# A diagonal of r·u·k made on VectorE in token order, in a linear-attention, MLP and soft-expert kernel

## What is computed

```python
# r, k, v, w: (batch 4, heads 8, seq 768, head_dim 48); u: (8, 48)
for t in range(S):
    kt, vt, rt, wt = (k[:, :, t], v[:, :, t], r[:, :, t], w[:, :, t])
    cur = np.einsum('bhd,bhe->bhde', u[None] * kt, vt)
    y[:, :, t] = np.einsum('bhd,bhde->bhe', rt, state + cur)
    state = wt[:, :, :, None] * state + np.einsum('bhd,bhe->bhde', kt, vt)
...
h = x @ w_in                                  # x: 3072 x 384, w_in: 384 x 2048
x = (h * (1.0 / (1.0 + np.exp(-1.702 * h)))) @ w_out
# then soft experts: phi 384 x 32, 8 experts, w1 384 x 1024, w2 1024 x 384 each
```

## Time and profile before

| | |
|---|---|
| time, median of 3 runs | 597.43 us (597.21 to 599.02) |
| profiled execution, its own time | 598.29 us |
| span of its trace | 596.6 us |
| granted TensorE clock, mean | 0.992 |
| PE busy | 573.4 us (96%), 6335 instructions |
| DVE busy | 329.6 us (55%) |
| ACT busy | 264.0 us (44%) |
| chain that ended last | PE 83%, DMA 7%, DVE 3%, issue 3%, ACT 2%, SP's queue 2% |

### The profile page before, as it was taken

The page is one execution under the profiler, slowest core; times in us unless marked ns, Lnnn a source line. Parts: engine busy times, 40 slices in busy tenths (PEclk is TensorE's granted clock), DMA queues, the critical chain, the costliest instruction groups (busy, mean ns, idle before and its releaser), DMA issues.

```text
span 596.6 us, 15329 instructions
## 1 busy us (share of the span) xinstructions
PE 573.4 (96%) x6335; PEld 523.4 (88%) x6335; DVE 329.6 (55%) x713; ACT 264.0 (44%) x540; POOL 10.5 (2%) x28
## 2 busy tenths in 40 slices
PE   8889999999999999999999999999999999999983
PEld 6788989889989998999999999999999999998332
DVE  8778777657846664566445645576364224323304
ACT  3955444363463335333544344333533356554313
POOL 4010000000000000000000000000000000000000
PEclk9999999999999999999999999999999999999996
DMA  8994523323432322222212322232111197768728
GB/s 282 381 221 161 150 79 102 90 79 89 110 97 73 87 70 63 63 66 84 87 50 87 88 57 78 73 88 73 56 48 27 40 387 243 230 223 280 245 77 317
DMA packets 52983, 77.52 MB, mean 130 GB/s; under 512 B 4256, under 2 KB 33440, under 8 KB 52576
## 3 DMA queue, kind: packets, MB, share of 16 engines
q1 hardware_dynamic: 41872, 54.88, 28.8%
q10 hardware_dynamic: 10240, 18.50, 10.1%
q0 software_dynamic: 800, 3.15, 1.7%
HBM read 67.46 MB, written 9.04 MB: 128 GB/s over the span
## 4 chain that ended last, share of the span: by engine, by line
PE 83%; DMA 7%; DVE 3%; issue 3%; ACT 2%; SPq 2%; ACTq 0%; DVEq 0%
PE hps L1417 33%; PE acc L1552 32%; DMA spare<-w_in 4%; DMA w2s<-w 2%; PE zps L1340 2%; PE mps L1358 2%; PE yps L1352 1%; PE mps L1451 1%; PE mps L1635 1%; PE zps L1352 1%; PE mps L1668 1%; PE zps L1346 1%; DMA out<-obuf 1%; PE mps L1648 1%; PE hps L1712 1%
## 5 line engine op out<-in xcount | busy, mean ns | idle before, releaser
L1185 DVE TENSOR_TENSOR gl<-g,gh 128x384 fp32r<-128x384 f32 (+1 forms) x144 | 73.9, 513 | 209.0 <-ACT gh L865 208.9
L1417 PE MATMUL hps<-xh,wi_hi 128*128 128x384 f32 (+1 forms) x432 | 146.8, 340 | 3.5 <-ACT g L854 2.2
L1417 PE MATMUL hps<-xh,wi_lo 128*128 128x384 f32 (+1 forms) x432 | 137.2, 318 | 0.0
L1417 PE MATMUL hps<-xl,wi_hi 128*128 128x384 f32 (+1 forms) x432 | 137.0, 317 | 0.0
L854 ACT ACTIVATE g<-hps 128x384 f32<-128x384 f32 (+1 forms) x144 | 65.6, 455 | 146.4 <-PE hps L1417 146.2
L1552 PE MATMUL acc<-wo_hi,gl 128*128 128x384 f32 x384 | 129.2, 337 | 0.0
L1552 PE MATMUL acc<-wo_lo,gh 128*128 128x384 f32 x384 | 129.2, 336 | 0.0
L1552 PE MATMUL acc<-wo_hi,gh 128*128 128x384 f32 x384 | 129.0, 336 | 0.2 <-issue 0.2
L865 ACT ACTIVATE gh<-g 128x384 fp32r<-128x384 f32 (+1 forms) x144 | 70.5, 489 | 118.1 <-PE acc L1552 117.5
L1417 PEld LDWEIGHTS hps<-xh,wi_hi 128*128 128x128 f32 x432 | 81.2, 188 | 13.7 <-issue 5.3
L1417 PEld LDWEIGHTS hps<-xl,wi_hi 128*128 128x128 f32 x432 | 81.5, 189 | 0.9
(11 more groups left out here) (251 smaller groups left out, 734.2 us busy)
## 6 DMA issues: line engine op xcount, KB each, us to landing
w1s<-w SPq DMA_DIRECT2D x16, 768.0 KB, 6.6
w2s<-w SPq DMA_DIRECT2D x16, 768.0 KB, 6.2
raw<-dmaj ACTq DMA_DIRECT2D x40, 225.8 KB, 2.6
vn<-vnat SPq DMA_DIRECT2D x24, 192.0 KB, 2.5
tests<-wall SPq DMA_DIRECT2D x6, 768.0 KB, 15.0
out<-obuf SPq DMA_DIRECT2D x12, 384.0 KB, 4.0
raw<-dmaj ACTq DMA_DIRECT2D x20, 226.2 KB, 2.5
raw<-dmaj ACTq DMA_DIRECT2D x20, 225.3 KB, 2.5
```

The lines of the kernel that those rows point to most:

```text
L1185: dve.tensor_tensor(out=gl[F % 2][:, 0:wide], in0=g32[F % 2][:, 0:wide], in1=gh[F % 2][:, 0:wide].bitcast(fp32), op=ALU.subtract).then_inc ...
L1417: last = pe.matmul(hps[F % 2][:, 0:wide], w[:, g, at:at + 128], v[i % 2][:, g, 0:wide], start=m == 0, stop=m == 3 * G - 1)
```

## The change

The bonus no longer goes through PE for n of 2 and more. r and k come a second time in token order (rknat, one load per block by ACT's queue, `load_n`, in place of the load of v's field; the first, for block 2, by SP), and v's field leaves raw. DVE's `weigh(n)` multiplies r·k, multiplies by u (u_row), and sums each head's 48 numbers: three instructions that wait for one another, giving b as a column of 8 numbers per token. `mask_scores(n)` first writes b times an identity (eye) over all of `scores` and then copies the PE scores over it where the mask is set, so the block's own output matmuls add b·v. The outputs then need no sum: ACT copies them from zps and yps to ybuf (`take_output`), for n = 0 and 1 DVE does (`first_output`). For n = 0 and 1 b still comes from PE, in matmuls with 2 columns. In the slot tables weigh stands at one slot where bonus_a and bonus_b were, some parts of blocks 2 to 4 move by a slot, and low_part(4) moves from slot 6 to behind the meeting of slot 5. SP issues raw 2 after the products of block 0 and not after bonus_values(0).

```diff
-        raw = [sb(f"raw{i}", [R, 4, HP, C + 1]) for i in range(2)]
+        raw = [sb(f"raw{i}", [R, NQ, HP, C + 1]) for i in range(2)]
...
-        ruk = [sb(f"ruk{i}", [R, HP, C]) for i in range(2)]
-        rukh = sb("rukh", [R, HP, C], f32r)
-        rukl = sb("rukl", [R, HP, C], f32r)
...
+        natural = sb("natural", [C, 2, DM])
+        u_row = sb("u_row", [C, DM])
+        bonus = [sb(f"bonus{i}", [C, H]) for i in range(2)]
...
-        place_parts(2, scan=1, invert=1, grow=2, decayed=3, bonus_a=4, turn=4, bonus=6)
-        place_parts(3, scan=5, invert=7, grow=7, turn=8, decayed=8, bonus_a=8, bonus=10)
-        place_parts(4, scan=13, invert=14, grow=15, turn=16, decayed=15, bonus_a=11, bonus_b=13, split=16, bonus=17)
...
+        place_parts(2, scan=1, invert=1, grow=2, weigh=3, decayed=3, turn=4, mask=8)
+        place_parts(3, load_n=5, scan=5, invert=6, grow=6, decayed=7, turn=8, weigh=9)
+        place_parts(4, load_w=7, load_k=9, load_r=10, load_n=11, scan=13, invert=14, grow=15, weigh=14, decayed=15, turn=16)
...
             n, f = BASE[i + 1] + 1, NF * i
-            place_parts(n, scan=f - 6, invert=f - 5, grow=f - 5, bonus_a=f - 3, bonus_b=f - 2, decayed=f - 1,
...
-            place_parts(n + 1, scan=f + 1, invert=f + 2, grow=f + 3, bonus_a=f + 4, bonus_b=f + 4, decayed=f + 5,
-                        turn=f + 5, split=f + 5, bonus=f + 6, load_w=f - 2, load_k=f - 1, load_r=f, load_v=f + 1)
+            place_parts(n, load_w=f - 8, load_k=f - 7, load_r=f - 6, load_n=f - 5, scan=f - 6, invert=f - 5, grow=f - 5,
+                        weigh=f - 2, decayed=f - 1, turn=f)
+            place_parts(n + 1, load_w=f - 2, load_k=f - 1, load_r=f, load_n=f + 1, scan=f + 1, invert=f + 2, grow=f + 3,
...
-        low_at = {0: 2, 4: 3, 6: 4, 9: 5, 10: 6, 12: 7}
+        low_at = {0: 2, 4: 3, 9: 5, 10: 6, 12: 7}
+        low_behind = {5: 4}
...
             for n in range(NCH):
                 if n < PRE:
-                    sp.wait_ge(uv_done, n + 1)
+                    sp.wait_ge(decayed_done, n + 1)
+                    sp.wait_ge(front, n + 1)
+                    sp.wait_ge(rk_made, n + 1)
                     load_raw(n + 2)
+                if n == 0:
+                    sp.dma_start(u_row[:, :], urow).then_inc(u_row_in, 16)
+                if n == 1:
+                    sp.dma_start(natural[:, :, :], rknat[PRE]).then_inc(rows_in, 16)
...
                 act.activation(kn[n % 2][:, :, :], mps[:, 0:HP * R].rearrange("t (p d) -> t p d", p=HP),
                                ACT.Copy).then_inc(kn_done, 1)
 
+            def take_output(n):
+
+                act.wait_ge(meetings, met_out[n])
+                if n >= 2 * PRE:
+                    act.wait_ge(y_stored[n % 2], 32 * (n // 2 - 1))
+                else:
+                    act.wait_ge(permuted, PRE)
...
+                    cols = slice(HALF * c, HALF * (c + 1))
+                    last = act.activation(ybuf[n % 2][:, :, cols], (zps, yps)[c][0:R, 0:HP * HALF].rearrange("e (p t) -> e p t", p=HP),
+                                          ACT.Copy)
...
-                if (F, "load_v") in part_at:
-                    n = part_at[F, "load_v"]
-                    act.wait_ge(uv_done, n - 1)
...
-                if (F, "split") in part_at:
-                    n = part_at[F, "split"]
...
-                    act.activation(rukh[:, :, :], ruk[n % 2][:, :, :], ACT.Copy).then_inc(rukh_done, 1)
+                if (F, "load_n") in part_at:
+                    n = part_at[F, "load_n"]
+                    act.wait_ge(weighed, 3 * (n - PRE))
+                    act.dma_start(natural[:, :, :], rknat[n]).then_inc(rows_in, 16)
                 if (F, "turn") in part_at:
                     turned_keys(part_at[F, "turn"])
+                if F in meeting_at and meeting_at[F][0] is not None:
+                    take_output(meeting_at[F][0])
...
-
-                if n == FULL and half == 0:
-                    dve.wait_ge(u_in, 16)
-                await_field(n, RR)
-                await_field(n, KK)
-                for p in (2 * half, 2 * half + 1):
-                    last = dve.scalar_tensor_tensor(ruk[n % 2][:, p, :], field(n, RR)[:, p], ucols[:, p:p + 1], field(n, KK)[:, p],
-                                                    ALU.mult, ALU.mult)
-                if half:
-                    last.then_inc(ruk_made, 1)
-
...
 
-                dve.tensor_tensor(out=ruk[n % 2][:, :, :], in0=field(n, RR), in1=field(n, KK), op=ALU.mult).then_inc(ruk_made, 1)
+                dve.tensor_tensor(out=rk[n][:, :, :], in0=field(n, RR), in1=field(n, KK), op=ALU.mult).then_inc(rk_made, 1)
...
+            def weigh(n):
+
...
+                dve.wait_ge(rows_in, 16 * (n - PRE + 1))
+                done = 3 * (n - PRE)
+                dve.tensor_tensor(out=natural[:, 0], in0=natural[:, 0], in1=natural[:, 1], op=ALU.mult).then_inc(weighed, 1)
+                dve.wait_ge(u_row_in, 16)
+                dve.wait_ge(weighed, done + 1)
+                dve.tensor_tensor(out=natural[:, 0], in0=natural[:, 0], in1=u_row[:, :], op=ALU.mult).then_inc(weighed, 1)
+                dve.wait_ge(weighed, done + 2)
+                dve.tensor_reduce(bonus[n % 2][:, :], natural[:, 0].rearrange("t (h d) -> t h d", h=H), AX, ALU.add).then_inc(weighed, 1)
 
             def invert(n):
...
             def mask_scores(n):
...
                 if n < PRE:
-                    dve.wait_ge(z_done, n + 1)
+                    dve.wait_ge(bonus_made, n + 1)
                 else:
-                    dve.wait_ge(meetings, met_in[n])
+                    dve.wait_ge(weighed, 3 * (n - PRE + 1))
+                weight = (acc[1][:, 0:H] if n < PRE else bonus[n % 2][:, :]).rearrange("t (p r) -> t r p", r=2)
                 if n and n <= PRE:
                     dve.wait_ge(av_done, n)
                 elif n:
                     dve.wait_ge(meetings, met_out[n - 1])
+                dve.tensor_tensor(out=scores[:, :, :, :], in0=eye[:, :].unsqueeze(1).unsqueeze(1).broadcast_to([C, 2, HP, HALF]),
+                                  in1=weight.unsqueeze(3).broadcast_to([C, 2, HP, HALF]), op=ALU.mult).then_inc(diagonal, 1)
+                if n < PRE:
+                    dve.wait_ge(z_done, n + 1)
+                else:
+                    dve.wait_ge(meetings, met_in[n])
+                    dve.wait_ge(y_done, n)
+                dve.wait_ge(diagonal, n + 1)
                 for par in range(2):
-                    dve.tensor_tensor(out=scores[:, par], in0=score_banks(n)[par].rearrange("s (p t) -> s p t", p=HP),
-                                      in1=mask[:, :].unsqueeze(1).broadcast_to([C, HP, HALF]),
-                                      op=ALU.mult).then_inc(scored, 1)
-
-            def bonus_values(n):
-
-                dve.wait_ge(u_done, n + 1)
-                await_field(n, VV)
-                if n >= 2 * PRE:
-                    dve.wait_ge(y_stored[n % 2], 32 * (n // 2 - 1))
-                elif n >= PRE:
-                    dve.wait_ge(permuted, PRE)
-                dve.tensor_tensor(out=ybuf[n % 2][:, :, :], in0=bonus_bank(n)[0:R, :].rearrange("e (p t) -> e p t", p=HP),
-                                  in1=field(n, VV), op=ALU.mult).then_inc(uv_done, 1)
+                    dve.copy_predicated(scores[:, par], mask[:, :].bitcast(i32).unsqueeze(1).broadcast_to([C, HP, HALF]),
+                                        score_banks(n)[par].rearrange("s (p t) -> s p t", p=HP)).then_inc(scored, 1)
...
-            def add_output(n):
...
-                    dve.wait_ge(meetings, met_out[n])
...
                 for c in range(2):
                     cols = slice(HALF * c, HALF * (c + 1))
-                    last = dve.tensor_tensor(out=ybuf[n % 2][:, :, cols], in0=(zps, yps)[c][0:R, 0:HP * HALF].rearrange("e (p t) -> e p t", p=HP),
-                                             in1=ybuf[n % 2][:, :, cols], op=ALU.add)
+                    last = dve.tensor_copy(ybuf[n][:, :, cols], (zps, yps)[c][0:R, 0:HP * HALF].rearrange("e (p t) -> e p t", p=HP))
                 last.then_inc(y_done, 1)
 
...
+                decays(1)
+                dve.wait_ge(eye_made, 1)
                 mask_scores(0)
-                decays(1)
                 first_state(0)
                 next_state(0)
                 invert(1)
                 decayed(1)
                 grown_keys(1)
-                bonus_values(0)
                 products(1)
-                add_output(0)
+                first_output(0)
...
-                bonus_values(1)
-                add_output(1)
+                first_output(1)
                 low_part(0)
                 bound_decays(0)
...
-                if (F, "bonus_a") in part_at:
-                    n = part_at[F, "bonus_a"]
-                    if n < FULL:
-                        products(n)
-                    else:
-                        bonus(n, 0)
-                if (F, "bonus_b") in part_at:
```

(32 more changed lines are left out.)

100 lines of the change are left out of this document (48 added, 52 removed).

## The result

The changed kernel takes **594.31 us** (median of 5 runs, 592.47 to 594.64) against 597.43 for the kernel before: ratio 0.9943, 95% interval 0.9926 to 0.9960. Run again later with six executions it gave 0.9935 (0.9915 to 0.9956). It is faster by 0.6%. The prediction was 588.6 us with a range of 584.6 to 592.6: the sign is right, the gain is about 3 us where 8.8 were forecast.

What follows compares the result with a forecast made beforehand. PE was taken as the bound from 300 to 400 us, with DMA engines fully busy from 10 to 40. Terms 9.2 + 1.0 - 1.4 = 8.8 us less than 597.43 gave 588.6 us, range 584.6 to 592.6.

Steps and rivals of the forecast that it cites:

- The pair of matmuls, 20 blocks: PE, blocks 4 to 23: removing rukh and rukl matmuls saves 0.46 us per block, 9.2 us in all.
- The starts of steps 2 and 3: Slots 32 and 48: weigh delays xl, so PE waits about 0.7 us each time, 1.4 us back.
- Step 4 on: Step starts from slot 64: 1.35 us of cover against 1.1 us of extra DVE work, so priced at nothing.
- weigh's price: DVE: two chained multiplies and a reduction, about 0.57 + 0.57 + 0.5 = 1.65 us.
- ACT: Behind each meeting: two output copies of 0.38 us each fit into ACT's idle time; priced at nothing.
- the rest of DVE: DVE work per block besides weigh, including predicated copies of 0.4 to 0.8 us; priced at nothing.
- The start-up ... I take 1.1: Before the first GELU: 452 KB less queued ahead of the load it waits for, so it starts 1.1 us earlier.
- Step 0 ... 1.0 us less: Slots 2 to 15: after weigh's extra DVE work, slot 16 starts 0.3 to 2.1 us earlier, taken as 1.0.
- the bonus sums of blocks 2 and 3: PE in step 0: their eight passes go, 0.79 us each block, 1.6 us together, counted within step 0's sum.
- Rivals: Four alternatives: boundaries and step 0 free, 0.19; DVE behind, 0.15; ACT limits PE, 0.03; pair's PE time not returned, 0.03.
- B: DVE falls behind in step 0, slot 16 starts 2.5 us later, later steps miss cover: 592.9 us, chance 0.15.
- The prediction is wrong if slot 16 comes later than 76.0: Sign of failure at the start of step 1: PE's slot 16 later than 76.0 us; about 75.0 was expected.

Runs made afterwards that it cites:

- e1_warm: Changed kernel plus two idle filling matmuls of 512 columns behind each of the bonus sums of blocks 0 and 1; 592.07 us, ratio 0.9907 to the kernel before.
- e3_both: Changed kernel plus two filling matmuls behind each bonus sum of blocks 0 and 1, and weigh one slot later ahead of steps 1 to 3; 589.07 us, ratio 0.9858.
- e4_nopair: Kernel before with the pair of 512-column matmuls of blocks 4 to 23 replaced by one of 32 columns, their bonus left out; 591.07 us, ratio 0.9894.
- e5_narrow: Kernel before with the bonus sums of blocks 0 and 1 cut to two columns, their bonus left out; 600.45 us, ratio 1.0024.
- e8_after_again: Changed kernel, unedited, run again; 593.83 us, ratio 0.9935 to the kernel before.

## Why the prediction was off, step by step

- **"The pair of matmuls, 20 blocks": right.** From slot 64 to slot 120 the eleven blocks give 5.10 us, 0.46 each, in both difference columns of the table.
- **"The starts of steps 2 and 3": right.** 0.75 and 0.76 us against 0.7, with the waits at the places named. **Step 4 on: right**, nothing lost.
- **weigh's price: right.** 1.69 us against 1.65; the parts 0.53, 0.56 and 0.55. The trace again shows chained instructions further apart (0.63 and 0.59 us) than one that does not wait for the one ahead (0.47). The Trainium skill, page "VectorE: DVE Perf Modes", section "The DRAIN you can't avoid", says that a semaphore after each costs nothing extra; these rows speak against it here too.
- **"ACT" and "the rest of DVE": right.** Copies of 0.39 and 0.38 us in idle time; predicated copies of 0.45 and 0.43, at the lower end of 0.4 to 0.8.
- **"The start-up ... I take 1.1": wrong, and the main miss.** The first hidden layer is 3.06 us later. With the clock kept (e1_warm) it is 0.78 us later, of which some 0.6 are the filling itself. VectorE's chain was near level, as forecast: kd of block 1 is 0.11 us later than before, and midway behind it, 0.47 later, waits for PE's state sums. The load of the earlier trace rows did let go of the chain: the conversion of the weights behind it no longer waits for it. But then the branch on the flag, which follows the bound sums on PE, ends last: flag at 33.76, the branch through at 35.47, the GELU at 35.62. With the clock kept the first GELU starts at 33.34, 0.38 us earlier than before (33.72), but PE starts slot 2 at 34.83, 1.11 us behind that GELU's end where it was 0.55 before; so nothing of the 1.1 us reached PE. The forecast priced the load that ended last and not the chain right behind it. The other 2.3 us of the first hidden layer are the clock: it was at 1.2 GHz for some 7 us between 18 and 26, behind passes that stream 2 columns in place of 128 and a pause. The prediction treated PE's time as fixed: that the bonus sums of blocks 0 and 1 become narrow does not stand in its sum at all, a term left at nothing without a reason. The later falls took as much again: the second 1.4 us (slots 2 to 5), the third 1.4 (slot 17). At slot 18 the changed kernel is 5.0 us behind e1_warm.
- **"Step 0 ... 1.0 us less": wrong.** Slot 16 starts 4.07 us late. 3.35 were there at slot 3. With the clock kept (e1_warm) it is 0.39 us late: 0.21 at slot 3, then 2.0 us gained by slot 9, where the bonus sums of blocks 2 and 3 were (1.6 forecast), then 2.17 lost again by slot 16. With weigh out of slot 14 (e3_both) only 0.48 are lost there. So weigh's place costs 1.7 us. From slot 15 to slot 16 alone the changed kernel loses 1.47 us where I had 1.1 for weigh less the half of ruk; e3_both gains 0.24 there, so what went there was worth 0.24 and not 0.52. What is lost besides, 0.5 us, has no term in the forecast: PE waits 0.86 us for the scores of block 3 in this stretch. The rows were not late: VectorE shows no wait for them. The fall of the clock that came with the 2.44 us of waiting took 1.4 us more by slot 18 (+4.07 to +5.00 in place of e1_warm's +0.39 to -0.04).
- **Not forecast, in the other direction:** between slots 26 and 27 the changed kernel gains 1.10 us. The profile before has a pause there that is put down to issue, as e4_nopair and e5_narrow have, and the one after has not:

```profile
110.11 0.56 PE L1358 MATMUL mps<-vn,kn 64*48 64x48 f32 x15 [0.90 <-issue]
```

- **Rivals.** B named step 0 as the place where it would be lost, "slot 16 starts 2.5 us later", but by late rows, weigh and copies; its time, 592.9, is nearest by luck: with the clock kept slot 16 is 0.39 us late and not 2.5, and of its causes only weigh shows. None of the rivals had the clock. "The prediction is wrong if slot 16 comes later than 76.0" was the sign to look for, and it came.

With the clock kept, the sum closes by other terms than forecast: e1_warm's profiled execution is 9.05 us under that of before (8.8 forecast), with +0.39 at slot 16 where -1.0 was forecast, against 1.1 us gained between slots 26 and 27 and 0.9 behind slot 120 that weren't. The changed kernel shows these two as well; what brings the second stays open. So the agreement with 588.6 is partly luck.

What stays open: what exactly lets the clock fall in one execution and not in the next. The runs show it behind a wait of PE of 1.3 to 2.4 us or behind narrow passes and a pause, and not behind each of them: the kernel before waits 2.17 us ahead of slot 2 and e1_warm 2.45 us ahead of slot 16, and neither profile shows a fall there. With the filling behind the bonus sums the mean granted clock is higher in each of three pairs (0.988 against 0.983, 0.991 against 0.988, 0.990 against 0.983), but one profile for each version cannot say which fall became rarer. That the narrow passes cause the first fall is thus likely and not proven: e8_after_again falls ahead of those of block 1, and a version of the changed kernel with wide bonus sums was not run. The pauses for issue were not tried by themselves.

## What to carry to other kernels

Read the granted clock of the start-up in short stretches, of several executions, before you take PE time away there: matmuls that stream little or a new wait of 2 us can cost more than the removed work was worth, and filling matmuls are worth it only where PE would stand still anyway and no branch or late result is behind them. When a chain loses its last link, price the next link before you book the gain. And work that is moved ahead of a split that the next step waits for costs time there; but look at what stands behind its new place too: one slot later weigh saved 1.7 us at the start of step 1 and nothing at that of step 2, where the next result in VectorE's order came late in place of the split.
